# Ready-made weight pairs kept in DRAM, copies ahead of casts and the first activations in two loads, in a kernel of windowed attention and two feed-forward layers

## The reference, cut to what matters

```python
# q, k, v: 4 batches, 8 heads, 576 tokens, 64 channels, float32
scores = scale * q @ k.T + bias;  masked to 0 <= i - j < 128
attn = softmax(scores) @ v
x = attn as (2304 tokens, 512)
h = x @ w_in;   y = (h * sigmoid(1.702 * h)) @ w_out      # layer one, w_in 512 x 2048, w_out 2048 x 512
h = y @ w_in2;  g = where(h >= 1, h, where(h <= -1, 0, (h + 1)**2 / 4))
out = g @ w_out2                                           # layer two, same sizes
```

## Time and profile before

| | |
|---|---|
| runs | 950.85, 950.94, 954.05 us, median 950.94 |
| the profiled execution | 949.0 us, span 947.2 us |
| PE busy | 886.7 us, 94% |
| VectorE (DVE) busy | 705.1 us, 74% |
| ACT busy | 547.3 us, 58% |
| POOL busy | 115.8 us, 12%, all of it in the attention |
| mean granted TensorE clock | 0.982 |
| chain that ended last | PE 69%, DVE 17%, issue 6%, ACT 4%, DMA 3% |
| HBM | 107.54 MB read, 61.34 MB written |
| first, small split of a pair (L1303) | 419 ns |

### The profile page before, as it was taken

How to read it: one execution, slowest core, us unless ns; L and a number is a source line. 1 busy time by engine, 2 the same in 40 slices (tenths; PEclk the granted TensorE clock), 3 DMA queues, 4 the chain that set the end, 5 groups by cost and what they waited for, 6 DMA issues and landing times.

```text
span 947.2 us, 16202 instructions
## 1 busy us (share of the span) xinstructions
PE 886.7 (94%) x5804; PEld 858.7 (91%) x5804; DVE 705.1 (74%) x1048; ACT 547.3 (58%) x946; POOL 115.8 (12%) x85
## 2 busy tenths in 40 slices
PE   5999979999999999999899999998899999987998
PEld 5999869899999999999899998998899999987998
DVE  5777766565587867655798788989787788986793
ACT  4777858566565445656633457674554567653531
POOL 3667877200000000000000000000000000000000
PEclk9999999999999999999999999998999999999999
DMA  9988782346356335384545562633643544436633
GB/s 216 231 213 212 173 239 83 124 181 246 110 194 239 123 134 204 128 323 169 203 162 189 200 232 102 256 122 123 242 160 112 189 172 172 166 124 221 242 125 113
DMA packets 55636, 169.81 MB, mean 179 GB/s; under 512 B 6672, under 2 KB 12688, under 8 KB 52496
## 3 DMA queue, kind: packets, MB, share of 16 engines
q1 hardware_dynamic: 55568, 168.90, 54.2%
HBM read 107.54 MB, written 61.34 MB: 178 GB/s over the span
## 4 chain that ended last, share of the span: by engine, by line
PE 69%; DVE 17%; issue 6%; ACT 4%; DMA 3%; SPq 1%; POOL 0%; DVEq 0%; ACTq 0%; POOLq 0%
PE ps L826 54%; DVE arena L1355 6%; PE ps L787 6%; PE ps L751 4%; PE ps L768 3%; ACT arena L1020 2%; DVE raw_first L1340 1%; DVE g L1384 1%; DMA ust<-zd 1%; DMA raw_first<-xd 1%; DVE w_rest L1305 1%; DVE raw_first L1349 1%; DVE wst L1298 1%; DVE raw_rest L1344 1%; PE ps L800 1%
## 5 line engine op out<-in xcount | busy, mean ns | idle before, releaser
L826 PE MATMUL ps<-arena,w_first 128*128 128x384 f32 x1764 | 336.5, 339 | 10.9 <-DVE ust L1452 2.9
L826 PEld LDWEIGHTS ps<-arena,w_first 128*128 128x128 f32 x1764 | 312.2, 189 | 16.6 <-issue 15.6
L826 PE MATMUL ps<-arena,w_rest 128*128 128x384 f32 x1260 | 243.7, 338 | 7.8 <-ACT d1s L1057 2.7
L1355 DVE TENSOR_TENSOR arena<-raw_first,arena 128x768 fp32r<-128x768 f32 (+1 forms) x116 | 151.1, 1313 | 111.6 <-ACT arena L1020 111.1
L826 PEld LDWEIGHTS ps<-arena,w_rest 128*128 128x128 f32 x1260 | 219.8, 188 | 13.2 <-issue 12.3
L1020 ACT ACTIVATE arena<-raw_first 128x768 fp32r<-128x768 f32 (+1 forms) x120 | 131.7, 1117 | 78.6 <-DVE raw_first L1340 49.1
L826 PE MATMUL ps<-w_rest,arena 128*128 128x256 f32 x945 | 136.5, 287 | 11.6 <-DVE ust L1412 5.7
L826 PEld LDWEIGHTS ps<-w_rest,arena 128*128 128x128 f32 x945 | 124.8, 195 | 12.3 <-issue 12.3
L826 PE MATMUL ps<-w_first,arena 128*128 128x256 f32 x567 | 90.6, 288 | 9.3 <-ACT ps L1065 4.9
L1020 ACT ACTIVATE arena<-raw_rest 128x1536 fp32r<-128x1536 f32 (+1 forms) x48 | 61.0, 1270 | 53.4 <-DVE raw_rest L1344 24.6
L826 PEld LDWEIGHTS ps<-w_first,arena 128*128 128x128 f32 x567 | 78.7, 195 | 9.9 <-issue 9.9
(11 more groups left out here) (84 smaller groups left out, 926.6 us busy)
## 6 DMA issues: line engine op xcount, KB each, us to landing
gd<-g SPq DMA_DIRECT2D x24, 1536.0 KB, 6.1
raw_rest<-gd SPq DMA_DIRECT2D x32, 768.0 KB, 6.8
qk_raw<-qkT SPq DMA_DIRECT2D x64, 288.0 KB, 5.1
wst<-w_pairs SPq DMA_DIRECT2D x32, 512.0 KB, 4.1
raw_first<-gd SPq DMA_DIRECT2D x16, 768.0 KB, 7.6
yd<-ust SPq DMA_DIRECT2D x6, 1536.0 KB, 6.3
raw_first<-xd SPq DMA_DIRECT2D x4, 1536.0 KB, 6.7
raw_first<-yd SPq DMA_DIRECT2D x4, 1536.0 KB, 6.4
```

What stands on the lines that cost most here:

```text
L826: last = nc.tensor.matmul(to, stationary, moving, start=start and n == 0, stop=n == len(steps) - 1, skip_group_check=True)
L1355: nc.vector.tensor_tensor(at[:, 1], source(k, i), f32(at[:, 0]), ALU.subtract).then_inc(lo_made, 1)
```

## The change

Pairs are now made in the order `MADE`, and even and odd are counted in that order (`nth`, `odd`). Eight pairs of layer two, `STOCK`, are made early and stored in DRAM (`wd`), then loaded whole into their slots when these are free: 18 and 19 are made in the attention (batches 0 and 1), 22 and 23 and 30 and 31 in down 0, 26 and 27 in down 2. So up 2 and up 3 make pairs only in chunk 0's second group and in chunk 1, and the other up work for pairs stays in phases 0 and 1. The stocks made in down stages are built in the tile `g`, so the store of the last one is waited for by ACT's C11 and VectorE's C22 of the next phase's first group. On ACT, `seed_b` and `copy_d` come ahead of the casts of an up or down group, `seed_c` ahead of the activation, and the pairs 8u + 6 and 8u + 7 are cast earlier. On VectorE S3 of the next down chunk is summed at the end of the group before, pair 8u + 3 is summed ahead of the split of S4, and pair 8u + 7 split ahead of C12. The first chunk's activations are loaded in two halves (tokens 0 to 383 at q = 9 of SP's attention loop, 384 to 767 at q = 13) in place of one load at q = 14.

```diff
+MADE = (18, 19, 0, 1, 2, 3, 4, 5, 6, 7, 8, 22, 9, 23, 30, 31, 10, 11, 12, 13, 14, 15, 16, 17, 20, 21, 24, 26, 25, 27, 28, 29)
+STOCK = (18, 19, 22, 23, 30, 31, 26, 27)
+DOWN_PAIRS = {(0, 0): (8, 22), (0, 1): (9, 23), (0, 2): (30, 31), (1, 0): (16,), (1, 1): (17,), (2, 0): (24, 26), (2, 1): (25, 27)}
+        def store_stock(w):
+            sp.wait_ge(w_ready, 3 * (nth(w) + 1))
+            sp.dma_start(wd[STOCK.index(w)], f32(w_made(w))).then_inc(w_stored[min(STOCK.index(w), 2)], 16)
+        def load_stock(w):
+            if STOCK.index(w) < 2:
+                sp.wait_ge(w_stored[STOCK.index(w)], 16)
+            else:
+                sp.wait_ge(w_stored[2], 16 * (stocks_in_g(w) + 1))
+            w_released(sp, w)
+            sp.dma_start(f32(w_place(w)), wd[STOCK.index(w)]).then_inc(w_loaded[w % W_SLOTS], 16)
...
         load_values(0, HEADS - 1)
+        load_weights(18)
+        load_weights(19)
...
             if q == 6:
+                store_stock(18)
                 load_weights(0)
-            if q == 8:
+            if q == 9:
+                load_first_x(0)
+                store_stock(19)
                 load_weights(1)
             if q == 13:
+                load_first_x(1)
                 load_weights(2)
-            if q == 14:
-                load_x(0, 0)
...
+        def up_transfers(u):
             load_x(u, 1)
+            if u >= 2:
+                load_stock(8 * u + 3)
+                load_stock(8 * u + 2)
             load_weights(8 * u + 4)
...
             load_hidden(u, 0, 0, 1)
+            if u >= 2:
+                load_stock(8 * u + 6)
+                load_stock(8 * u + 7)
+            if u < 3:
                 load_weights(8 * u + 8)
             store_hidden(u, 2, 0)
...
+            if u < 3:
                 load_x(u + 1, 0)
+            if u == 0:
+                store_stock(pairs[2][0])
+                load_weights(10)
                 store_y(u, 2)
+                store_stock(pairs[2][1])
+                load_weights(11)
```

On POOL (the steps run behind the split of head h):

```diff
+        def during_first(h):
+            if h == 5:
+                add_weights(18, 0)
+            if h == 6:
+                add_most_weights(18)
+            if h == 7:
+                split_weights(18, 0)
+        def during_second(h):
+            if h in (0, 1):
+                split_weights(18, h + 1)
+            if h == 2:
+                add_weights(19, 0)
+            if h == 3:
+                add_most_weights(19)
+            if h in (4, 5, 6):
+                split_weights(19, h - 4)
```

On ACT, an up group (first of a chunk) and the down group:

```diff
             seed_b(D, 0)
-            if c == 0:
-                round_operand(k, S3)
-                seed_b(D, 1)
+            seed_b(D, 1)
+            if c == 0 and u < 2:
                 round_weights(w + 2, 0)
-                copy_d(D, 0)
+            copy_d(D, 0)
+            round_operand(k, S3)
+            if c == 0 and u < 2:
                 round_weights(w + 2, 1)
-                seed_c(D)
-                round_operand(k, S4)
-                copy_d(D, 1)
-                round_operand(k, A22)
+            seed_c(D)
+            copy_d(D, 1)
+            round_operand(k, S4)
+            round_operand(k, A22)
+            if c:
+                activate(u, c - 1, 1)
+            elif u < 2:
                 round_both(w + 3)
...
+            pairs = DOWN_PAIRS.get((u, c), ())
+            seed_b(D, 0)
             round_operand(k, A12)
-            seed_b(D, 0)
             seed_b(D, 1)
+            copy_d(D, 0)
             round_operand(k, S3)
-            copy_d(D, 0)
+            if pairs:
+                round_both(pairs[0])
+            seed_c(D)
             if c == 0:
                 activate(u, CHUNKS - 1, 1)
-            if c < 2 and u < PHASES - 1:
-                round_both(8 * u + 8 + c)
-            seed_c(D)
...
+            if len(pairs) > 1:
+                round_both(pairs[1])
             if u % 2 == 0:
                 down_c21(u, c)
```

On VectorE, an up stage and the down group:

```diff
             split_operand(k, S3)
-            if c == 0:
+            if c == 0 and u < 2:
                 split_weights(w + 2)
+                add_weights(w + 3)
             split_operand(k, S4)
             if c == 0:
-                add_weights(w + 3)
                 up_c22(u, c, 0)
                 split_operand(k, A22)
-                split_weights(w + 3)
+                if u < 2:
+                    split_weights(w + 3)
...
             if c == 2:
-                split_weights(w + 6)
-                add_weights(w + 7)
+                if u < 2:
+                    split_weights(w + 6)
+                    add_weights(w + 7)
+                split_operand(k + 1, A11)
                 up_c22(u, c, 1)
-                split_operand(k + 1, A11)
                 if u >= 2:
                     larger(u, c, 0)
+                else:
+                    split_weights(w + 7)
                 up_c12(u, c, 1)
-                split_weights(w + 7)
                 split_operand(k + 1, S1)
                 sum_operand(k + 1, S2)
+                sum_operand(k + 1, S3)
                 split_operand(k + 1, S2)
...
-            sum_operand(k, S3)
             sum_operand(k, S4)
             split_operand(k, A12)
+            if pairs:
+                add_weights(pairs[0])
             split_operand(k, S3)
+            if pairs:
+                split_weights(pairs[0])
             if u >= 2 and c == 0:
                 larger(u, CHUNKS - 1, 1)
-            if more:
-                add_weights(w + c)
             split_operand(k, S4)
             split_operand(k, A22)
...
             down_c22(u, c)
             if not last:
                 sum_operand(k + 1, S1)
-            if more and c < 2:
-                split_weights(w + c)
+            if len(pairs) > 1:
+                add_weights(pairs[1])
...
             if u % 2:
                 add_c21(u, c)
+            if len(pairs) > 1:
+                split_weights(pairs[1])
+            if not last and c < 2:
+                sum_operand(k + 1, S3)
             if not last:
                 split_operand(k + 1, S2)
                 if c == 2:
                     split_operand(k + 1, A12)
+            if u == 0 and c == 2:
+                add_weights(10)
```

More of the change, by code:

```diff
@@ L184, in build @@
     w_ready = sem("w_ready")
+    w_stored = [sem("w_stored_first"), sem("w_stored_second"), sem("w_stored_g")]
+    w_loaded = [sem(f"w_loaded{i}") for i in range(W_SLOTS)]
+    x_first = [sem("x_first_top"), sem("x_first_bottom")]
     x_in = [sem("x_in_even"), sem("x_in_odd")]
@@ L569, in _ @@
             store_pair(q)
-        for u in range(PHASES):
-            more = u < PHASES - 1
+        def up_transfers(u):
             load_x(u, 1)
+            if u >= 2:
+                load_stock(8 * u + 3)
+                load_stock(8 * u + 2)
             load_weights(8 * u + 4)
@@ L602, in _ @@
             load_hidden(u, 1, 0, 0)
+            if len(pairs[0]) > 1:
+                load_weights(pairs[1][0])
             load_hidden(u, 1, 0, 1)
-            if more:
-                load_weights(8 * u + 10)
             load_hidden(u, 2, 1, 1)
@@ L624, in _ @@
                 store_last_y()
+        for u in range(PHASES):
+            up_transfers(u)
+            down_transfers(u)
         sp.wait_ge(y_stored, 16 * (PHASES * CHUNKS + 2))
@@ L844, in product_1 @@
             pe.wait_ge(lo_made, OPS * k + A11 + 1)
-            weights_ready(u, up, c, D, pos, P1)
+            if up and c == 0:
+                weights_ready(8 * u + 2 * (D % DUOS % 2) + pos)
+            if not up and c == 0 and n == 0:
+                for w in range(8 * u + PAIRS, 8 * u + 2 * PAIRS):
+                    weights_ready(w)
             wait_past(pe, c21_out, D - 1 + n)
@@ L899, in first_products @@
                 pe.wait_ge(lo_made, A11 + 1)
[L900 removed]
+                weights_ready(0)
                 mark_written(3)
```

245 lines of the change are left out of this document (151 added, 94 removed).

## The result

The kernel after takes **966.5 us** (median of 4 runs, 964.3 to 966.9), the kernel before beside it 952.5 (4 runs). The ratio is **1.014** (95% interval 1.011 to 1.017): 1.4% slower, where 943.4 us, faster, was forecast and the range ended at 956. Its profiled execution took 966.5 us, span 964.7, mean clock 0.972.

What follows compares the result with a forecast made beforehand. TensorE, busy 94% of the span, was taken as the bound, only idle time and slow matmuls winnable. 949.0 - 3.4 (attention) - 21.0 (stage gains) + 16.9 (transfers) = 941.5; with 1.9, 943.4 us; range 921 to 956.

Steps and rivals of the forecast that it cites:

- The halves: Attention: loading the first activations in halves removes ACT's stall for them, 12.93 - 4.82 = 8.1 us gained.
- Pair 18: Attention: POOL's sum of pair 18 waits for its load ahead of head 6's split; 3.8 us lost, bounds 0 and 5.
- The stores of the pairs: Attention: the pairs' stores (1792 KB) and halves' waits on SP have over two heads of lead; nothing lost, at worst 1 us.
- What the copies give: Stages: ACT's copies ahead of casts, earlier weights, VectorE's new order and fewer slow matmuls take PE's waits away; 21.0 us gained.
- VectorE is the bound of the down stages: Rival, 18%: with two more pairs per group row in down 0 and down 2, groups come late, 6 us in all; 949.
- 21.6 us free: Argument against the VectorE rival: in down 0 VectorE has 91.3 - 69.7 = 21.6 us free for 7 us more work.
- Up 1: Start of up 1: pair 11's load lands late behind two stores, then VectorE's sum and split; 5.3 us lost.
- The weights at the start of down 2 and down 3: Layer two's two "issue" waits for down-stage weights, 8.7 us, go; 6.4 counted as gained, the new loads just in time.
- Up 2 and up 3: Starts of up 2 and up 3: two ready-made pairs land behind chunk 1's load; 4.4 and 6.2 us lost.
- The clock: Stages: slow matmuls that follow the new idle time, 1.0 us lost.
- The pairs travel slowly: Rival, 12%: ready-made pairs' loads take 2.1 us more each, 17.5 on top; 960.9 us, slower than before.
- The cover holds: Rival, 25%: loads overtake what is ahead, or VectorE was not waiting there; the 3.8 and 16.9 losses go; 922.7 us.

Runs made afterwards that it cites:

- run 1: Kernel before plus only the first activations loaded in two halves, with ACT's first two casts of them moved; 946.3 us, ratio 0.995.
- run 14: run 5 without the store of pair 19 (wrong values in layer two), ACT's rounding of pair 1 waiting for pair 19's split alone; 944.1 us.
- run 3: Kernel after with only pairs 18 and 19 ready-made, in the attention, the six others made in place; 954.7 us, ratio 1.004.
- run 5: run 3 with POOL's work for pairs 18 and 19 two heads later and both their stores later; 949.5 us.
- run 6: run 3 with the store of pair 19 and load of pair 1 issued behind the loads of heads 20 and 21; 949.7 us.
- run 2: Kernel after without any ready-made pair; halves, ACT's copies ahead of casts and VectorE's new order stay; 936.0 us, ratio 0.985.
- run 9: run 2 with VectorE's split of the next down chunk's S2 ahead of the sum of its S3; 936.6 us, ratio 0.984.
- run 10: run 9 with, in layer two, S4's split (down) and the last weight pair's split (up) ahead of the larger-of; 939.3 us, ratio 0.987.
- run 11: run 4 with VectorE's split of S2 ahead of the second pair's split and of S3's sum; 949.8 us.
- run 7: run 4 with stores copying a pair that stands still, so ACT need not wait for them before the next pair (wrong values); 946.2 us.
- run 4: Kernel after with only the six pairs made in down 0 and down 2 ready-made, 18 and 19 made in place; 950.8 us, ratio 1.002.

## Why the prediction was wrong

The forecast was -7.5 us against the median of before; +14.0 came. By the profiled executions (-7.5 predicted, +17.5 measured) 8.5 of the 25 lie in the attention and 16.5 in the stages.

- **The halves, -8.1.** Right in kind, mis-sized: -5.5 (run 1). The step that failed is "heads otherwise follow each other by 4.82", taken from heads 6 and 7, where POOL has nothing but their splits to do and stands idle 1.9 us a head. With its weight and activation steps POOL fills 5.28 us a head, and in before's own trace the casts just ahead of the stall were already 5.21 to 5.24 us apart. "What is late next is listed here" was carried out for the pairs and not for the halves themselves. The cast beside a busy POOL takes 1.69 us against 0.75 in each of these heads. The lock on a shared port that the Trainium skill describes (SBUF — State Buffer, "SBUF: two separate sides") points this way, and the trace agrees with the direction; but POOL's and ACT's whole work for two pairs cost 2.7 us (run 14) where 0.9 was taken and the 4 us more would have made 4.9.
- **Pair 18, +3.8.** Right in place and kind (POOL idle 6.70 us before its sum, the load landing at 34.2 for a predicted 36.0), mis-sized: 7.0 in run 3, above the bound of 5. Head 6 itself came only 2.6 us late, PE's wait was 2.4. The failed step is that the wait was taken for the whole loss: the fall of the clock behind it was put at nothing in the attention and cost the larger part.
- **The stores of the pairs, "nothing, at worst 1 us".** Wrong, and with pair 18 the dearest step in the attention: 5.3 us at heads 20 and 21, of them 2.0 PE's wait and the rest slow matmuls. The bound came from the heads' lead on SP, but the store, the half load and the next pair's load stand in one queue ahead of a head's load, 11.3 us to landing (runs 5, 6, 14).
- **What the copies give, 21.0.** L1049, L1057, "issue" and L1065, which was to stay, went; L1068 went with the pairs, but 3.4 of its 3.6 us are there in run 2; of L1452's 2.9, 1.9 are left in both. Run 2's profile has 4.4 us of gain in its stages, and the medians of runs 1 and 2 (946.3 and 936.0), less the 1.1 us between their first products, give 9.2, where 14.6 (without the 6.4 that need the pairs) had been counted. The step that failed is the sum of waits taken as time gained: only for chunk 1's waits did it ask what comes next, and the answer given there (VectorE's split) held everywhere, 12.5 us. The rival that VectorE is the bound of the down stages had the nearest mechanism at 18%: runs 9, 10 and 11 move its waits and do not remove them. Against it stood "21.6 us free" in down 0, a mean over the stage; the group of chunk 1 has 31.6 us of VectorE's work in its 29.5.
- **Up 1, +5.3.** 8.8 came (excess 10.5 against 1.7). Failed step: "the wait of ACT and VectorE for pair 31's store hides in it". It looked at the guard at the end of the chain and not at the one between pairs: pair 30's cast waits for pair 23's store, pair 31's for pair 30's (run 7).
- **The weights at the start of down 2 and down 3, 6.4 of the 21.0.** Failed step: the loads of 22, 23, 30 and 31 "just in time, 0 to 1". PE's 8.6 us of waiting for pairs made too late (7.3 in run 2) became 7.0 for pairs landed too late (3.7 and 3.3): 16.5 us from issue to landing in a group of 14.8. The time of what stood ahead in the queue was assumed at 4 us, and took 7 to 8.
- **Up 2 and up 3, +4.4 and +6.2.** Right: the two pairs land 5.3 and 4.3 us behind chunk 1 in up 2, 4.3 and 4.3 in up 3; with runs 3 and 4 against run 2, the first two groups lose 4.3 and 5.9 us. Slow matmuls are in these sizes, some 1.3 us of the 4.3, which the prediction has in its next term, so the sizes are in part luck.
- **The clock, +1.0.** Far too small, and taken for the stages alone: 4.4 us in up 1's first group, 7.9 in run 3's attention.
- **Rivals.** "The pairs travel slowly" gave the nearest time, 960.9, by a mechanism that the traces do not bear out: 1792 KB landed 4.2 to 5.8 us behind what was ahead of it, for the 4.5 assumed and the rival's 6.6. 1792 KB in 4.30 us are 427 GB/s. The 358 GB/s that the Trainium skill (DMA: Bandwidth & Descriptors, "Bandwidth") has as the limit for transfers between HBM and SBUF, and as each core's part when both cores of a pair stream, do not bound this kernel on its one core. "The cover holds" fell with the landings in order of issue.

## What to carry to other kernels

A wait taken away is worth the distance to the next one in line, on every engine; list that next wait for each term before adding it up, and do not take a pace from heads in which an engine has less to do than in those that the change touches. When work is moved, look for the areas it shares (here one tile through which six pairs pass, each held until its store has landed) and for the queue its transfers stand in; a 1792 KB store ahead of small, urgent loads cost 5.3 us here, and 8.0 in another place, more than its own 4.3 of transfer. Price a wait with the slow matmuls behind it: 2.4 us of waiting cost 7.0. Take the parts of a change apart: this one held a gain of 1.5% and a loss of 2.9%.

## What was not expected of the hardware

After 3.6 us without a matmul the granted clock was 0.50 for the next 4 to 5 us of work, so a wait of 3.6 us cost some 6; in the attention it was 0.50 for 9.8 us after a wait of 2.4 (run 3). It does not follow from the length of the wait alone: behind the same wait of 2.95 us in down 0 it was 1.00 in the kernel after and 0.55 in run 4. Loads and stores of one queue landed in the order of issue, a load behind a store as much as behind a load (11.3 us for 288 KB). The start of the attention scatters between executions: the step from head 2 to head 3 was 4.4 us in one profile and 8.0 in three others with the same code up to there, the runs of one kernel spread over up to 11 us, and single profiles of two kernels are not to be compared by less than some 4 us.
